# Weight loads of an attention kernel issued every second step instead of every fourth, two of them from another queue

## What is computed

```python
def reference(q, k, v, n_global, n_local, moe_phi, moe_w1, moe_w2, moe2_w_in, moe2_w_out):
    # q, k, v: (4, 8, 768, 64). Attention: causal window of n_local=96 keys and the first n_global=8
    # keys, with a bias that falls with distance; softmax over the kept keys; times v
    x = attn_ref(q, k, v, n_global, n_local)        # -> (3072, 512)
    # soft mixture of experts: phi (512, 32), w1 (8, 512, 1024), w2 (8, 1024, 512)
    logits = x @ phi
    d = softmax(logits, axis=0)                     # over the 3072 tokens, for each of 32 slots
    slots = (d.T @ x).reshape(8, 4, 512)
    out = [relu(slots[e] @ w1[e]) @ w2[e] for e in range(8)]
    x = softmax(logits, axis=1) @ concat(out)
    # second layer: w_in (512, 2048), w_out (2048, 512)
    return relu(x @ w_in) ** 2 @ w_out
```

## Time and profile before

| | us |
|---|---|
| median of 3 runs | 526.86 (526.18 to 527.32) |
| the profiled execution, its own time | 526.18 |
| span of the profiled execution | 524.4 |
| TensorE busy in the span | 487.9 (93%) |
| ScalarE busy | 345.6 (66%) |
| VectorE busy | 364.6 (70%) |
| GpSimd busy | 94.7 (18%) |
| first to last exponentials of attention | 12.95 to about 189 |

### The profile page before, as it was taken

One profiled execution on the slowest core, in us unless ns is written; L12 is line 12 of the kernel. 1 busy time (PEld: TensorE's weight loads), 2 busy tenths in 40 slices (PEclk: granted clock), 3 DMA queues, 4 the chain that ended last, 5 costly groups with the idle time before them and its releaser, 6 DMA issues.

```text
span 524.4 us, 12778 instructions
## 1 busy us (share of the span) xinstructions
PE 487.9 (93%) x4573; PEld 399.4 (76%) x4573; DVE 364.6 (70%) x1027; ACT 345.6 (66%) x758; POOL 94.7 (18%) x223
## 2 busy tenths in 40 slices
PE   2799999999999998789899999999999999999997
PEld 1566666666666653223689999999999999999996
DVE  5586676777667765222798997777776777768783
ACT  1678878777777751002898987677776777777750
POOL 1454454445444423300000000000000000000000
PEclk9799999999999999989999999999999999999999
DMA  6779889886544389999201010110101101011011
GB/s 244 273 258 355 310 293 302 270 328 229 192 150 137 140 292 392 387 391 386 75 1 41 1 42 1 41 40 0 40 0 40 40 0 40 0 40 40 0 41 41
DMA packets 24587, 77.24 MB, mean 147 GB/s; under 512 B 2528, under 2 KB 2528, under 8 KB 21984
## 3 DMA queue, kind: packets, MB, share of 16 engines
q1 hardware_dynamic: 19680, 60.96, 31.9%
q10 hardware_dynamic: 4864, 15.73, 8.4%
HBM read 70.39 MB, written 6.29 MB: 146 GB/s over the span
## 4 chain that ended last, share of the span: by engine, by line
PE 62%; ACT 10%; DVE 9%; POOL 6%; issue 5%; DMA 3%; SPq 3%; ACTq 0%; DVEq 0%; POOLq 0%
PE bank L1541 14%; PE bank L1540 14%; PE bank L1542 14%; ACT probs L965 9%; POOL probs L426 6%; PE bank L1512 4%; SPq L376 3%; PE bank L1221 3%; DMA wo_raw<-w_out_dram 3%; DVE probs L517 2%; PE bank L1261 2%; PE bank L1466 1%; PE bank L1446 1%; PE bank L1248 1%; PE bank L1559 1%
## 5 line engine op out<-in xcount | busy, mean ns | idle before, releaser
L965 ACT ACTIVATE probs<-probs,nmax 128x232 f32<-128x232 f32 (+1 forms) x192 | 88.6, 462 | 49.4 <-DVE nmax L517 49.3
L426 POOL TENSOR_SCALAR probs<-probs,rden 128x232 f32<-128x232 f32 (+1 forms) x192 | 82.7, 451 | 104.4 <-DVE rden L526 104.4
L1540 PE MATMUL bank<-t_hi,s_hi 128*128 128x256 f32 x352 | 98.7, 280 | 0.0
L1541 PE MATMUL bank<-t_lo,s_hi 128*128 128x256 f32 x352 | 98.6, 280 | 0.0
L1542 PE MATMUL bank<-t_hi,s_lo 128*128 128x256 f32 x352 | 98.5, 280 | 0.0
L1088 ACT ACTIVATE g_s<-bank 128x1024 f32<-128x1024 f32 x48 | 49.0, 1023 | 30.5 <-PE bank L1512 30.5
L1117 ACT ACTIVATE s_hi<-s 128x512 fp32r<-128x512 f32 x88 | 55.1, 627 | 19.1 <-DVE s L900 14.6
L1221 PE MATMUL bank<-ident,probs 128*128 128x128 f32 x352 | 56.5, 289 | 11.5 <-POOL probs L426 10.1
L1540 PEld LDWEIGHTS bank<-t_hi,s_hi 128*128 128x128 f32 x352 | 66.5, 189 | 0.0
L1541 PEld LDWEIGHTS bank<-t_lo,s_hi 128*128 128x128 f32 x352 | 66.4, 189 | 0.0
L1542 PEld LDWEIGHTS bank<-t_hi,s_lo 128*128 128x128 f32 x352 | 66.4, 189 | 0.0
(11 more groups left out here) (192 smaller groups left out, 1007.6 us busy)
## 6 DMA issues: line engine op xcount, KB each, us to landing
qkv_s<-qkv_dram SPq DMA_DIRECT2D x16, 1028.0 KB, 6.7
qkv_s<-qkv_dram SPq DMA_DIRECT2D x16, 704.0 KB, 4.1
w_s<-w_dram ACTq DMA_DIRECT2D x5, 2048.0 KB, 10.6
w_s<-w_dram SPq DMA_DIRECT2D x15, 512.0 KB, 8.7
out_dram<-o_stage SPq DMA_DIRECT2D x24, 256.0 KB, 2.0
w_a<-w_dram SPq DMA_DIRECT2D x9, 512.0 KB, 7.0
wo_raw<-w_out_dram SPq DMA_DIRECT2D x4, 1024.0 KB, 13.7
w_pre<-w_dram ACTq DMA_DIRECT2D x1, 2048.0 KB, 11.1
```

What stands on the lines that cost most here:

```text
L426: last = pool.tensor_scalar(probs[:, v % 2, m, a, 0:w], probs[:, v % 2, m, a, 0:w], rden[:, v % 2, m, a:a + 1], 1.0, ALU.mult, ALU.mult)
L965: act.activation(probs[:, v % 2, m, a, 0:w], probs[:, v % 2, m, a, 0:w], ACT.Exp, bias=nmax[:, v % 2, m, a:a + 1], scale=-1.0, accum_out=d ...
L1540: pe.matmul(OUT[n], hi, W_HI[n](at_f), start=(c == 0 and f == 0 and n in (0, 2, 4, 5)), stop=False, skip_group_check=True)
L1541: pe.matmul(OUT[n], hi, W_LO[n](at_f), start=False, stop=False, skip_group_check=True)
```

## The change

The eight transfers stay what they are: same tiles, same sources, same semaphores. Six are still issued by ScalarE, but after the turns for steps 1, 3, 5, 7, 9 and 11, so that all six are issued in the first batch. The other two are now SP's: `w1_c` follows `load_v(2, 1)` and `win_c[0]` follows `load_v(4, 1)`. The branch that the kernel takes with these inputs is the one called `windowed`.

```diff
@@ sync (SP)
                     for n in range(2):
                         ...
                         load_v(k, n)
+                    if k == 2:
+                        sp.dma_start(w1_c[:, :, :], w1_v[4]).then_inc(w1_c_in, 16)
+                    elif k == 4:
+                        load_win(2)
@@ scalar (ACT)
-                def load_early(n):
-                    if n < 4:
-                        act.dma_start(w1_s[n][:, :, :], w1_v[n]).then_inc(w1_in[n], 16)
-                    elif n == 4:
-                        act.dma_start(w2_s0[:, :, :], w2_v[0]).then_inc(w2_in[0], 16)
-                    elif n == 5:
-                        act.dma_start(w2_pre[:, :, :], w2_v[1]).then_inc(w2_in[1], 16)
-                    elif n == 6:
-                        act.dma_start(w1_c[:, :, :], w1_v[4]).then_inc(w1_c_in, 16)
-                    elif n == 7:
-                        act.dma_start(win_c[0][:, :], w_in[2 * P:3 * P, :]).then_inc(win_in, 16)
                 for s in range(STEPS):
                     step(0, s, False)
-                    if s % 4 == 0:
-                        load_early(s // 4)
+                    if s % 2 == 1:
+                        if s < 8:
+                            act.dma_start(w1_s[s // 2][:, :, :], w1_v[s // 2]).then_inc(w1_in[s // 2], 16)
+                        elif s == 9:
+                            act.dma_start(w2_s0[:, :, :], w2_v[0]).then_inc(w2_in[0], 16)
+                        elif s == 11:
+                            act.dma_start(w2_pre[:, :, :], w2_v[1]).then_inc(w2_in[1], 16)
                 for b in range(1, BATCH):
                     for s in range(STEPS):
                         step(b, s, True)
-                        if s % 4 == 0:
-                            load_early((b * STEPS + s) // 4)
```

## The result

The changed kernel took 530.59 us (median; 530.13 to 531.10), the kernel before 527.09 us beside it. The ratio is 1.0067, with a 95% interval of 1.0048 to 1.0088: slower by 3.5 us, where 0.9 us had been forecast and 529.6 was the top of the range. Why one kernel has two such times is part of the answer.

The account below looks back on a forecast made before the run. Attention's pace was taken as set by the ring between the engines (TensorE busy 41.9 of 44.35 us), not by loads. Nothing gained, 0.9 us lost to late qk(3,0): median 526.86 to 527.8 us, range 526.2 to 529.6.

Parts of the forecast that it names:

- none held: Rival: ScalarE's issue of `w2_pre` at 53.8 is held by a full queue, delaying exponentials 2 to 3 us; 530.5, chance 0.05.
- paid in full: At `scores(18)`, TensorE takes work in order, so lateness of qk(3,0) past 76.56 us delays everything behind it.
- Steps 1 to 4: Count of bytes on both queues from 19.2 us until qk(3,0) is moved behind `w1_c`: last byte at 76.7 us.
- my 395: Rate in GB/s taken for both queues together in attention's dense stretch, from measured 413, 402, 390 and 369.
- step 3: By 62.9 us 17.3 MB moved: SP's 6.4, ScalarE's 10.9 of 12.6, so 1.7 MB still to come.
- Step 4: From 62.9 us, SP's 3.87 MB through qk(3,0) with 1.57 MB of ScalarE's between: 13.8 us, last byte at 76.7.
- Step 5: Adds 1.0 us from last byte to landing of qk(3,0): 77.7, 1.1 us after TensorE's need at 76.56.
- the 0 to 2.1: Bounds in us on how late qk(3,0) lands for `scores(18)`, around the forecast 0.9.
- The sum: Count of whether `w1_c` and the denser ScalarE queue use up qk(3,0)'s 6.6 us margin: 0.9 us late.
- within 0.2%: Whole kernel: a change under 1.05 us, not told from none by a measurement; chance 0.54.

Follow-up runs that it names:

- e1: Changed kernel with `w1_c` issued right behind qk(3,0) instead of right ahead of it: 526.85 us, ratio 1.0008 to the kernel before.
- e2: SP's part of the change alone; ScalarE issues its six loads after turns 0, 4, ..., 20 as before: 526.87 us, ratio 1.0007.
- e3: ScalarE's part of the change alone; `w1_c` and `win_c[0]` issued by ScalarE after turns 24 and 28 as before: 527.12 us, ratio 1.0007.
- e5: Kernel before with twelve 128x128 products on TensorE put in front of `scores(18)`: 530.09 us, ratio 1.0066.
- e13: The changed kernel itself, unedited, measured and profiled a second time: 528.83 us, ratio 1.0038 to the kernel before.

## Why the prediction failed

**Right.** That nothing could be gained: e1, e2 and e3, which keep the sparse or the dense loads without the wait, are all within 0.08% of the kernel before. That ScalarE's issues cost nothing: six of 0.37 to 0.44 us, none held, the one of `w2_pre` at 53.88 (53.8 forecast). That qk(3,0) behind `w1_c` is the place, that a delay there is paid in full (e5), and that the other inputs stay in time: v(3,0) took 10.0 us and landed at 80.0.

**Steps 1 to 4** held in their result. By 62.9 us SP's queue had moved 6.37 MB and ScalarE's 10.90 (6.4 and 10.9 in step 3). The dense stretch ran at 405 GB/s, above my 395. Queues from 62.9 to 76.7 in the changed kernel (packets, MB, share; q1 is SP's):

```profile
q1 hardware_dynamic: 833, 4.00, 72.3%
q10 hardware_dynamic: 787, 1.59, 30.6%
```

Step 4 had 1.57 MB of ScalarE's between 3.87 MB of SP's, by 76.7. It is 1.59 and 4.00.

**Step 5 was too small.** The bytes were on time: SP's queue had moved 3.87 MB by 76.4, where 76.7 was forecast. But the landing came at 78.3, and by then the queue had moved 4.60 MB, 0.73 beyond qk(3,0). So most of the 16 engines were done with qk(3,0) and well into the next load, while the semaphore still wanted its last increments. The trace has their times: the first of the sixteen at 76.30, the eighth at 76.84, the last at 78.28. In the kernel before they are 69.01, 69.48 and 69.92. I took 1.0 us for the end from there; here it was 1.9 us. How long the queues had been full doesn't explain it: in e3 and e1, with the same dense stretch, the landing of qk(3,0) came 1.0 and 1.3 us behind its bytes, and in e2, where the core had moved only 278 GB/s from 20 to 62, it came 1.9 us behind. Common to e2 and the change is `w1_c` ahead in the same queue. Why the engines finish further apart behind it is open; the rows don't name the engines. The landing was 0.6 us later than forecast and TensorE's turn 0.2 earlier, so the wait became 1.94 us in one profile, and 1.61 in the other, instead of 0.9: inside the 0 to 2.1 that I had given, but not where I put it.

**The step that is missing is the clock.** The sum charges a late qk(3,0) with the length of its wait ("paid in full") and puts nothing beside it; it has no term for TensorE's clock, and no reason for leaving it out. Yet the trace of before shows a fall: 6.8 us at half clock, which begin within the one long idle stretch that TensorE has in attention after its first products. That was the sign that a new idle stretch could bring another. The fall costs 2.5 us: batch 3 begins 4.3 us later, 4.5 against the turns before the wait, and 2.0 of that are the wait. It alone carries the result over the top of my range: 530.59 less 2.5 is 528.1. Where it didn't come, in e13, the time of 528.83 lies in the range, and is 2.0 us above the kernel before where 0.9 had been forecast; 1.6 of that are the wait. So the loss was mis-sized twice over, by a tail and by a price that was not in the sum, and the forecast "within 0.2%" was wrong in both measurements. That the second measurement lies in the range is no merit of the sum: whether the clock falls was not in it.

What stays open: what, beside the idle stretch, decides whether the clock falls, since 1.6 and 1.9 us in one kernel and 4.5 us at the start have come out both ways; and what makes the expert stage's clock differ between executions.

## What to carry to other kernels

A load that nobody needs soon should stand behind the next one that somebody needs, not ahead of it. A second queue adds no room of its own, since both share the engines: qk(3,0) took 13.9 us behind `w1_c`, and 16.5 when ScalarE's queue was dense as well. When loads are moved, the margin to look at is the landing of each needed load against its first use, counted with all the bytes that are in flight ahead of it and with the tail of the landing (1.0 to 1.9 us here). And price a wait of TensorE in the middle of steady work as a range, from its length to its length and a fall of the clock (1.4 to 2.6 us more here). Look for the fall in the clock row of the profile that you start from.

## What the runs showed of the hardware

- TensorE's granted clock fell to half at the end of one wait of 1.9 us in steady work and stayed there for 6.8 us, but not at one of 1.6 in the same kernel; it fell within waits of 4.4 and 5.1 us. The price was 2.6, 1.4 and 2.1 us on top of the wait.
- One and the same idle stretch of 4.5 us near the start of the program brought a fall of 6.8 us in 6 of 16 profiles and none in 10.
- With 2 MB of another load ahead in its queue, the last increments of a 1.05 MB load came 1.9 us after as many bytes as lay up to its end had moved, with 0.73 MB of the next load already in; without it, 1.0 to 1.3 us, however long the queues had been full.
- The expert stage ran at a mean clock of 0.76 or 1.00 between 215 and 236 us in two executions of one kernel, with spans of 527.6 and 525.2. Of these 2.4 us, 1.7 arose there.
- Moving one of two tiny constant loads to a second queue ended the waits for the constants and for the input behind them 1.0 us later.
